# Sixteen attention pairs on one core: the diagonal blocks' empty quarter left out of scores and values

## The reference

```python
k_min, k_max = min and max of k over each chunk of 32 keys
ub = sum over features of max(q * k_min, q * k_max)       # a bound for each query and chunk
ub = where(chunk is not after the query's own, ub, -1e9)
sel = the 6 chunks with the largest ub, for each query
scores = where(sel and key <= query, q @ k.T / 8, -1e9)
attn = softmax(scores);  attn_out = attn @ v
```

## Time and profile before

| what | us |
|---|---|
| median of 3 runs | 266.8 (266.58 to 266.86) |
| the profiled execution, its own time | 266.53 |
| its span, first to last instruction | 264.8 |
| PE busy in the span | 256.2 |
| DVE busy | 213.2 |
| POOL busy | 211.3 |
| ACT busy | 149.6 |

### The profile page before, as it was taken

One profiled execution on the slowest core, in us unless ns is written; L12 is line 12 of the kernel. 1 busy time (PEld: TensorE's weight loads), 2 busy tenths in 40 slices (PEclk: granted clock), 3 DMA queues, 4 the chain that ended last, 5 costly groups with the idle time before them and its releaser, 6 DMA issues.

```text
span 264.8 us, 9133 instructions
## 1 busy us (share of the span) xinstructions
PE 256.2 (97%) x3824; PEld 164.4 (62%) x3824; DVE 213.2 (81%) x582; ACT 149.6 (56%) x227; POOL 211.3 (80%) x280
## 2 busy tenths in 40 slices
PE   7799999999999999999999999999999999989993
PEld 7366566666666566666665666656665657676763
DVE  6886696778989988867889889899999998983332
ACT  2295656565667564647584546564856665873320
POOL 6068889998999899897989898979899971726872
PEclk9999999999999999999999999999999999999999
DMA  9989989999799989997999999999799996941782
GB/s 147 189 145 149 235 225 261 228 187 224 125 208 180 209 145 195 173 219 125 215 160 215 171 190 164 215 162 324 142 207 184 328 212 142 165 103 40 136 167 91
DMA packets 148616, 48.34 MB, mean 183 GB/s; under 512 B 131583, under 2 KB 138870, under 8 KB 148512
## 3 DMA queue, kind: packets, MB, share of 16 engines
q1 hardware_dynamic: 135504, 28.73, 54.1%
q0 software_dynamic: 9936, 18.64, 38.6%
q10 hardware_dynamic: 3136, 0.39, 1.0%
HBM read 57.03 MB, written 11.01 MB: 257 GB/s over the span
## 4 chain that ended last, share of the span: by engine, by line
PE 91%; DVE 3%; ACT 2%; DMA 1%; issue 1%; ACTq 1%; POOL 0%; DVEq 0%
PE OB L637 28%; PE SC L546 27%; PE SC L567 7%; PE OB L1395 4%; PE MM L673 4%; PE SC L1369 4%; PE MM L650 3%; PE OB L721 2%; PE MM L474 2%; PE SC L474 2%; PE MM L513 2%; DMA qn<-in_q_dram 1%; ACT EXB L576 1%; PE MM L712 1%; PE MM L982 1%
## 5 line engine op out<-in xcount | busy, mean ns | idle before, releaser
L576 ACT ACTIVATE EXB<-SC 128x1024 f32<-128x1024 f32 (+1 forms) x87 | 83.1, 966 | 35.6 <-PE SC L546 23.9
L602 POOL TENSOR_TENSOR ES<-ES,EXB 128x512 f32<-128x512 f32 (+1 forms) x81 | 84.4, 1044 | 5.1
L546 PE MATMUL SC<-qT,kT 64*128 64x512 f32 (+3 forms) x476 | 86.3, 464 | 0.1
L637 PE MATMUL OB<-EXB,vn 128*64 128x256 f32 (+3 forms) x704 | 72.9, 361 | 0.0
L637 PEld LDWEIGHTS OB<-EXB,vn 128*64 128x64 f32 x704 | 46.1, 137 | 24.0 <-issue 10.4
L546 PEld LDWEIGHTS SC<-qT,kT 64*128 64x128 f32 x476 | 39.2, 187 | 15.8 <-issue 11.5
L602 POOL TENSOR_TENSOR ES<-EXB 128x512 f32<-128x512 f32 (+1 forms) x29 | 45.3, 1561 | 2.4
L586 POOL TENSOR_SCALAR_AFFINE_SELECT EXB<-EXB 128x256 f32<-128x256 f32 x79 | 34.9, 452 | 5.0 <-ACT EXB L576 5.0
L645 ACT ACTIVATE oT<-OB 128x512 f32<-128x512 f32 (+1 forms) x32 | 15.7, 490 | 40.1 <-PE OB L637 40.1
L567 PE MATMUL SC<-unsT,ind 64*128 64x256 bf16 (+5 forms) x238 | 35.6, 295 | 0.1
L567 PEld LDWEIGHTS SC<-unsT,ind 64*128 64x128 bf16 x238 | 11.8, 95 | 15.9 <-issue 7.1
(11 more groups left out here) (270 smaller groups left out, 405.0 us busy)
## 6 DMA issues: line engine op xcount, KB each, us to landing
w1s<-in_moe_w_dram POOLq DMA_DIRECT2D x8, 1024.0 KB, 8.6
w2s<-in_moe_w_dram POOLq DMA_DIRECT2D x7, 1024.0 KB, 13.9
vn<-in_v_dram SPq DMA_DIRECT2D x32, 192.0 KB, 4.5
kn<-in_k_dram SPq DMA_DIRECT2D x62, 96.0 KB, 3.2
qn<-in_q_dram SPq DMA_DIRECT2D x62, 96.0 KB, 3.5
out_dram<-w1s SPq DMA_DIRECT2D x2, 1536.0 KB, 7.2
out_dram<-out_dram SPq DMA_DIRECT2D x2, 1536.0 KB, 9.8
x_rows<-xp SPq DMA_DIRECT2D x7, 384.0 KB, 3.9
```

The lines of the kernel that those rows point to most:

```text
L546: op("pe", lambda: pe.matmul(o, kT[j][pr, ts(kt)], qT[j][pr, q0:q1], start=not flags and (not cols or cols[0] == 0), stop=bool(flags)), r= ...
L576: op("act", lambda: ac.activation(Ex(st, None, 0, W), src, ACTF.Exp, scale=SCALE), r=pk, w=[f"E{st}"])
L602: op(e, lambda: sy.queue[e].tensor_tensor(o, in0, in1, ALU.add), r=[f"E{s2}", f"E{first[0]}"] if first else [f"E{s2}"] + kt, w=kt)
L637: op("pe", lambda: pe.matmul(OB[pr, q0:q1], vn[s][:, kt, h, :], ex, start=(n == 0), stop=last), r=[f"vn{s}{h}", "ES0" if st is None else f ...
```

## The change

For pairs 1 to 14 ("turned"), the quarter of a diagonal block that holds its upper 64 keys and its lower 64 queries is left out, in key tiles 2 to 5. All of that quarter lies above the diagonal.

In scores, such a piece is issued as four matmuls with stationary tiles of 64 rows by 64 columns: for each key half and head, one. The key half that has the quarter streams 64 columns less. In key tiles 4 and 5 the two key halves change places in the partitions, so there the short half lies in partitions 0 to 63, and in 64 to 127 in key tiles 2 and 3. To keep pieces of both sorts next to one another, steps 3 and 4 issue their pieces in reverse. Flags of the exchanged tiles are issued in four matmuls too.

In values, the first 64 queries of a diagonal block only use the 64 lower keys. These come as matmuls with 64 x 64 stationary tiles, 64 columns long, two from different partition halves behind one another (a couple): (0, 5) with (1, 7), and in short pairs (0, 6) with (1, 8). In the other turned pairs only key tiles 2 and 4 are cut in values.

The exchanged key order needs v in the same order. So each v load of a turned pair becomes three transfers: key tiles 0 to 3, and two of 64 partitions for key tiles 4 and 5. POOL's select of an exchanged diagonal block becomes two instructions of 128 elements. The constant NEGSEL, which marks chunks after the query's own, goes from -1.0e9 to -3.0e38.

```diff
+    AVS_CUT = [
+        AVS[0][:3] + [(2, 320, 512, 2, 64), (3, 448, 512, 4, 64), (2, 256, 320, 2, 0), (3, 384, 448, 4, 0)],
+        AVS[1][:4] + [(4, 576, 768, 3, 320), (3, 512, 768, 4, 128), (5, 704, 768, 5, 64), (4, 512, 576, 3, 256), (5, 640, 704, 5, 0)],
+    ]
+    CUT_ORDER = [(0, 0), (0, 1), (0, 2), (0, 3), (1, 0), (1, 1), (1, 3), (0, 4), (0, 5), (1, 7), (0, 6), (1, 8), (1, 2), (1, 4), (1, 5), (1, 6)]
...
+                RT = 4
+                def turned(i):
+                    return 0 < i < NP - 1
...
+                        n = RT if turned(i) else NT
                         for h in range(2):
-                            a = bass.AP(src.tensor, src.offset + base + h * S * D, [[D, 128], [128 * D, NT], [1, D]])
-                            o = dst[s][:, :, h, :]
+                            a = bass.AP(src.tensor, src.offset + base + h * S * D, [[D, 128], [128 * D, n], [1, D]])
+                            o = dst[s][:, 0:n, h, :]
...
+                            for u in range(2 if n < NT else 0):
+                                a = bass.AP(src.tensor, src.offset + base + h * S * D + (n * 128 + (1 - u) * 64) * D, [[D, 64], [128 * D, NT - n], [1, D]])
...
+                        if turned(i) and st > 1 and q0 == kt * 128:
+                            r = int(kt >= RT)
+                            for u in (r, 1 - r):
+                                cut = 64 if u != r else 0
+                                for h in range(2):
+                                    pr = slice(h * 64, h * 64 + 64)
+                                    o = ps[u * 64:u * 64 + 64, pb + h * 512 + c + cut:pb + h * 512 + c + q1 - q0]
+                                    k0 = kt * 128 + (u ^ r) * 64
+                                    op("pe", lambda: pe.matmul(o, kT[j][pr, k0:k0 + 64], qT[j][pr, q0 + cut:q1], start=not flags, stop=bool(flags)),
...
+                        if turned(i) and st in (3, 4):
+                            pieces.reverse()
...
+                    if turned(i) and st in (3, 5):
+                        for u in (1, 0):
+                            x = a[0:64, :, 64:128] if u else a[:, :, 0:64]
+                            op("gp", lambda: gp.affine_select(x, x, pattern=[[0, 2], [1, 64]], compare_op=ALU.is_ge, fill=0.0,
+                                                              base=0 if u else 64, channel_multiplier=-1), r=[f"E{st}"], w=[] if u else [ak])
...
+                        if turned(i) and q1 - q0 == 64 and q0 == kt * 128:
+                            kp = slice(64, 128) if kt >= RT else slice(0, 64)
...
-                            op("pe", lambda: pe.matmul(OB[pr, q0:q1], vn[s][:, kt, h, :], ex,
+                            op("pe", lambda: pe.matmul(OB[pr, q0:q1], vn[s][kp, kt, h, :], ex[kp, :],
```

More of the change, by code:

```diff
@@ L11 @@
 AX = mybir.AxisListType.X
-NEGSEL = -1.0e9
+NEGSEL = -3.0e38
 MASKV = -65536.0
@@ L550, in scores, with flags @@
                     j = i % 2
-                    sts = (5, 4) if short(i) and hi == 6 else range(lo, hi)
-                    for st, pieces in [(n, STEPS[n]) for n in sts]:
+                    def flags(st, pi, first, inc):
+                        kt, q0, q1, c = STEPS[st][pi]
                         ps, pk = bank(i, st)
-                        pb = place(i, st)
-                        for pi, (kt, q0, q1, c) in enumerate(pieces):
-                            last = pi == len(pieces) - 1
-                            early = i > 0 and st == 2 or i > 0 and st == 4 and not short(i)
-                            if not early and (i or st > 2):
-                                score_mm(i, st, pi)
-                            if st == 0 and short(i):
-                                rows(i - 1)
-                            b0 = max(q0, 6 * CHUNK)
-                            assert not early or b0 == q0
+                        b0 = max(q0, 6 * CHUNK)
+                        assert not first or b0 == q0
+                        r = int(turned(i) and kt >= RT)
+                        c0 = place(i, st) + c + b0 - q0
+                        c1 = place(i, st) + c + q1 - q0
+                        cut = turned(i) and st > 1 and q0 == kt * 128 and not first
+                        halves = r or cut
+                        for u in range(2 if halves else 1):
+                            x = 64 if cut and u != r else 0
@@ L564, in scores @@
                             for h in range(2):
                                 pr = slice(h * 64, h * 64 + 64)
-                                o = ps[:, pb + h * 512 + c + b0 - q0:pb + h * 512 + c + q1 - q0]
-                                op("pe", lambda: pe.matmul(o, ind[pr, ts(kt)], unsT[j][pr, b0 - 128:q1 - 128],
-                                                           start=early, stop=not early),
-                                   r=[f"ind{h}", f"unsT{j}"] + (["unsTb"] if i == 0 and st else []), w=pk, inc=last and not early)
@@ L570, in scores @@
-                            if early:
-                                score_mm(i, st, pi, flags=True, end=last)
-                        if i == 0 and st == 2:
-                            short_warm()
-                        W = pieces[-1][3] + pieces[-1][2] - pieces[-1][1]
-                        src = bass.AP(ps, pb, [[1024, 128], [512, 2], [1, W]])
+                                ot = slice(u * 64, u * 64 + 64) if halves else slice(0, 128)
+                                k0 = kt * 128 + ((u ^ r) * 64 if halves else 0)
@@ new lines, in flags, with out @@
+                                op("pe", lambda: pe.matmul(ps[ot, h * 512 + c0 + x:h * 512 + c1], ind[pr, k0:k0 + (64 if halves else 128)], unsT[j][pr, b0 - 128 + x:q1 - 128],
+                                                           start=first, stop=not first),
+                                   r=[f"ind{h}", f"unsT{j}"] + (["unsTb"] if i == 0 and st else []), w=pk, inc=inc)
+                    def out(st):
+                        ps, pk = bank(i, st)
+                        W = STEPS[st][-1][3] + STEPS[st][-1][2] - STEPS[st][-1][1]
+                        src = bass.AP(ps, place(i, st), [[1024, 128], [512, 2], [1, W]])
@@ L581, in scores @@
                             folds(i, st)
+                    if short(i) and hi == 6:
+                        flags(5, 0, True, False)
+                        score_mm(i, 5, 0, flags=True, end=True)
+                        out(5)
+                        score_mm(i, 4, 0)
+                        flags(4, 0, False, False)
+                        score_mm(i, 4, 1)
+                        flags(4, 1, False, True)
+                        out(4)
+                        return
+                    for st in range(lo, hi):
+                        pieces = list(range(len(STEPS[st])))
+                        opens = [False] * 2
+                        if i and st == 2 or turned(i) and st == 5:
+                            opens[0] = True
+                        if i and st == 4 and not short(i):
+                            opens = [True] * 2
+                        if turned(i) and st in (3, 4):
+                            pieces.reverse()
+                        if turned(i) and st == 3:
+                            opens[1] = True
+                        for pi in pieces:
+                            last = pi == pieces[-1]
+                            if not opens[pi] and (i or st > 2):
+                                score_mm(i, st, pi)
+                            if st == 0 and short(i):
+                                rows(i - 1)
+                            flags(st, pi, opens[pi], last and not opens[pi])
+                            if opens[pi]:
+                                score_mm(i, st, pi, flags=True, end=last)
+                        if i == 0 and st == 2:
+                            short_warm()
+                        out(st)
                 def select(i, st):
```

20 lines of the change are left out of this document (16 added, 4 removed).

## The result

| | before | after |
|---|---|---|
| median, us | 266.8 (266.6 to 267.3) | 302.8 (298.0 to 307.7), 4 runs each |
| ratio of times | 1 | 1.124, 95% interval 1.111 to 1.137 |
| profiled execution, its span, us | 264.8 | 301.9 |
| 14 stretches from unselT of pair 1 to unselT of pair 15, us | 190.57 | 222.51 |

The ratio is taken over the runs within 1.5% of each kernel's fastest one (after the change 298.0 and 302.0 us).

The account below looks back on a forecast made before the run. PE, busy for 97% of the span, was taken as the bound. PE's +6.5 us and +0.4 for loads made +6.9 on 266.53, so 273.4, or 273.7 us in the median's terms; 80% range 271.0 to 277.3.

Parts of the forecast that it names:

- A change of shape: On PE, each change of the stationary tile's shape was priced at 0.095 us in which nothing streams.
- weights in the open: On PE, the first piece behind a shape change loads weights unhidden: 0.10 us for 128 float32 columns, 0.05 for 64.
- columns: On PE, streaming 64 float32 columns was priced at 0.108 us, 64 bfloat16 columns at 0.03.
- the four parts: PE's net cost a pair: scores +0.38 us (short pair) and +0.27 (other), values +0.09 and +0.19.
- The staggered starts: On PE, if four tiles stagger their starts, some 0.03 us more for each of three runs, +1 us.
- Four tiles side by side, the short half ahead: In scores, four 64*64 tiles stream together and a short half runs ahead; two pieces with opposite short halves save 0.108 us.
- halves in step: Rival, chance 0.12: in scores each four tiles wait for the longest, so scores save nothing; +2.9 us, 276.6.
- POOL costs nothing: POOL's split selects add 0.36 us a pair (0 to 0.72), but 0.33 of room remains before values: no cost.
- Weights hidden: Rival, chance 0.04: on PE only the drain at shape changes is paid; +1.8 and +0.4 us, 269.0.
- faster: Rival, chance 0.07: 64*64 counts as the same shape as tiles around it, no change is paid; 261.5 us.
- Loads: v comes in 6 transfers a pair, not 2 [...] hidden in the loop: SP issues 2.3 us more a pair; v, loaded 26 us ahead and landing in 4.5, costs nothing in the loop.
- Pair 0: Four more v transfers ahead of pair 2's q delay PE's unselT, less 1.44 us of room: 0.4 us (0 to 0.87).

Follow-up runs that it names:

- e5_act_late: Changed kernel with v's four small transfers issued from ACT's queue, behind rq of the pair before their use: 274.5 us, 1.030 of the kernel before.
- e2_two_loads: Changed kernel with v of each pair in two whole transfers as before, key halves of v not exchanged: 276.1 us, 1.024 of the kernel before.
- e4_store_act: Changed kernel with only the store of x_rows moved from SP's to ACT's queue, behind the exponentials of steps 4 and 5: 295.5 us, 1.064.
- e3_act_queue: Changed kernel with v's four small transfers issued from ACT's queue instead of SP's, ahead of the copy to unsT: 312.9 us.
- e13_store_behind_qk: Kernel before with only the store of x_rows moved on SP's queue, from ahead of the eight q and k loads to behind them: 296.3 us.
- e8_before_act: Kernel before with v of pairs 2 to 15 issued whole from ACT's queue behind rq of the pair before, not SP's: 276.0 us.

## Why the prediction was wrong, point by point

- **A change of shape, weights in the open, columns: right.** +0.47 and +0.46 a pair were forecast, 0.53 and 0.52 measured in pairs 3 and 7 (0.40 to 0.53 in the 14 pairs); over 14 stretches 6.9 us (e5_act_late) for 6.5. Each of the four parts is about 0.03 too low. The staggered starts, which I had only put into the range, are of that size; no run separates them.
- **Four tiles side by side, the short half ahead: right.** The flags at 59.55 start before the long half has streamed, so *halves in step* falls. On this the page TensorE: Matmul & The Clock Gate of the Trainium skill, Part 3, The mechanism, has matmuls start and end in order; the trace agrees for the first records, which start as issued (58.73 to 58.75); but the second records of the short half start at 59.17, ahead of those of the long half at 59.21, which is issued earlier, and the flags at 59.55 start while the long half still streams. With halves of unequal length neither starts nor ends are in order here.
- **POOL costs nothing: right.** In e2_two_loads and e5_act_late PE waits for POOL nowhere. *Weights hidden* and *faster* fall with the measured pairs.
- **"Loads: v comes in 6 transfers a pair, not 2 [...] hidden in the loop": the step that failed.** I held a lead of 26 us for v against 4.5 us to landing, and added 2.3 us of SP a pair without asking what SP had left, or what stands behind those issues. The lead was shorter: v has two buffers, so its load for pair i + 2 stands behind the values of pair i, and in the kernel before it is issued 12 to 20 us before its use (pairs 2 to 14). For pair 8 it lands 2.0 us ahead (122.72, used at 124.73). The 4.5 us are a median; the longest was 16.3. SP had little left: issues that begin between 25 and 213 us add up to 167.2 of the 188 us. At the free 0.58 its 137 issues would be some 79 us, by my estimate; the rest is time in which issues were held, up to 6.84 us for one load of v, which the price of a free issue leaves out. And SP's queue holds more than loads: the store of x_rows, which the prediction does not name, had a slack of 4.3 us ahead of the weights, and the change used it up. In pairs 5 and 13 it landed 13.8 and 14.7 us after issue, and scale_rows with all behind it waited; these two pairs hold 20.7 of the 37.1 us. In pair 5 v was nearly as late as the store, and with the store out of the way v was what PE waited for (e4_store_act).
- **Pair 0: the right place, the wrong size.** 0.4 us (0 to 0.87) were forecast, 2.8 measured. q's last issue ended at 18.79, 2.7 us later than before (I let v's transfers soak up part; they soaked up nothing and were held themselves, 2.49 us for two). And q landed 3.5 us after that, where before it took at most the 2.04 us to take_q. 2.7 and 1.5, less the 1.44 of room, is 2.8.

What stays open: why SP's issues are held beside the weights, for up to 6.8 us in the kernel before, 8.3 in the changed kernel and 3.3 in e3_act_queue, while ACT's 52 issues in the loop of that last run took 0.6 to 0.9 us; and what makes the 2 us by which the part behind the loop differs between runs.

## What to carry to other kernels

Before adding transfers to a queue, add up the time in which its engine already issues, stage by stage, and list everything that stands behind the new issues, stores too: the lead of the transfer itself says nothing about them. Count the time in which issues are held, not only their free price, and read the lead from the trace, from issue to use. For each store that frees a buffer, find the bulk transfer that starts next and the slack between the two. Where that slack is a few microseconds, another engine's queue at a place where that engine waits anyway is a cheap cure: here it made the kernel before steady (0.993 of its time on that chip). In the changed kernel the same move was not enough, since v came late as well.

## What the runs showed of the hardware that was not expected

- A few tenths of a microsecond in the place of a transfer among bulk transfers can cost 10 us. The same 384 KB store took 4.0 and 6.4 us when issued 0.8 us ahead of 2 MB of weights, and 14.6 to 15.2 us when issued 0.1 to 0.6 us behind a weight load (e13_store_behind_qk). The place alone does not settle it: in pair 13 of the changed kernel it took 14.7 us though it was issued 1.5 us ahead of the weights, behind a 1.5 MB copy.
- The issue of one and the same kind of transfer took 0.60 to 0.91 us on ACT in the loop of e3_act_queue and from 0.60 to 4.84 us on SP in the changed kernel. ACT's queue is not free of it: a whole load of v was held there for 5.65 us in e8_before_act.
- 64*64 tiles side by side go on half by half: in the changed kernel the next flags start 0.376 us behind the second records of 448 columns and 0.429 us behind those of 512, each on its own, though the long half is issued first.
